# Attention scores as four 64x64 TensorE tiles of two head pairs, with thirds-wise loads, in a fused attention and mixture-of-experts kernel

## The reference

```python
# q, k, v: (4 batches, 8 heads, 576 positions, 64)
scores = scale * np.matmul(q, k.transpose(0, 1, 3, 2))
mask = (rel >= 0) & (rel < 64)                 # rel = query position - key position
attn = softmax(np.where(mask, scores, -1e9))   # with 1e-09 added to the sum
x = np.matmul(attn, v)                         # rows: 2304 tokens x 512

x = ((x @ w1) * (x @ w2)) @ w3 @ w_out         # 512 -> 1024 -> 1024 -> 512

e_idx = argmax(x @ w_gate)                     # one of 8 experts per token
out[mask] = gate_w * sigmoid(x @ w_output_gate)[e] * (relu(x @ ew1[e]) @ ew2[e])
```

## Time and profile before

| | |
|---|---|
| Three timed runs | 757.87, 755.08, 758.03 us (median 757.87) |
| The profiled execution | 755.37 us, its span 753.6 us |
| TensorE busy / its weight loads | 722.7 us (96%) / 663.5 us (88%) |
| VectorE, ScalarE, GpSimd busy | 326.3 (43%), 297.9 (40%), 122.0 us (16%) |
| DMA | 80.08 MB in 64187 packets, 23501 of them under 512 B |

### The profile page before, as it was taken

How to read it: one execution, slowest core, us unless ns; L and a number is a source line. 1 busy time by engine, 2 the same in 40 slices (tenths; PEclk the granted TensorE clock), 3 DMA queues, 4 the chain that set the end, 5 groups by cost and what they waited for, 6 DMA issues and landing times.

```text
span 753.6 us, 14552 instructions
## 1 busy us (share of the span) xinstructions
PE 722.7 (96%) x4832; PEld 663.5 (88%) x4833; DVE 326.3 (43%) x641; ACT 297.9 (40%) x720; POOL 122.0 (16%) x191
## 2 busy tenths in 40 slices
PE   5999999999999999999999994999999999999994
PEld 5999999999999999999999994888888888888883
DVE  3577445412144524442221276736265544652120
ACT  3577444422045434443211242335345544542211
POOL 7012011200011111111000001112222221222111
PEclk9999999999999999999999996999999999999998
DMA  9985212420012241205101043446265654411110
GB/s 300 232 261 164 75 33 62 118 70 1 29 47 60 60 130 33 60 29 197 70 1 43 1 182 112 144 149 200 95 206 194 235 181 135 166 33 42 31 42 29
DMA packets 64187, 80.08 MB, mean 106 GB/s; under 512 B 23501, under 2 KB 43981, under 8 KB 64144
## 3 DMA queue, kind: packets, MB, share of 16 engines
q1 hardware_dynamic: 59104, 64.01, 27.6%
q0 software_dynamic: 5040, 15.47, 5.9%
HBM read 70.03 MB, written 10.49 MB: 107 GB/s over the span
## 4 chain that ended last, share of the span: by engine, by line
PE 93%; DVE 3%; DMA 1%; ACT 1%; issue 1%; POOL 0%; POOLq 0%; ACTq 0%; DVEq 0%
PE bank L428 26%; PE bank L430 25%; PE bank L429 25%; PE bank L478 5%; PE bank L499 3%; PE bank L598 2%; PE bank L488 2%; PE bank L578 1%; DMA xs<-x_rows,gid 1%; DVE wbuf L901 1%; PE bank L440 1%; PE bank L570 0%; PE bank L466 0%; PE bank L462 0%; DMA w3r<-in_w3T 0%
## 5 line engine op out<-in xcount | busy, mean ns | idle before, releaser
L428 PE MATMUL bank<-Wh,abh 128*128 128x272 f32 (+1 forms) x288 | 83.8, 291 | 0.0
L430 PE MATMUL bank<-Wh,abl 128*128 128x272 f32 (+1 forms) x288 | 82.1, 285 | 0.0
L429 PE MATMUL bank<-Wl,abh 128*128 128x272 f32 (+1 forms) x288 | 81.8, 284 | 0.0
L650 ACT ACTIVATE prob<-prob,nmx 128x128 f32<-128x128 f32 x144 | 56.3, 392 | 63.7 <-DVE nmx L820 63.7
L901 DVE TENSOR_TENSOR wbuf<-raw,wbuf 128x1024 f32 (+1 forms) x64 | 75.4, 1221 | 11.9 <-ACT wbuf L715 11.7
L1144 POOL TENSOR_TENSOR prob<-prob,rec 128x384 f32<-128x384 f32 x48 | 39.8, 828 | 217.8 <-DVE rec L830 217.8
L428 PE MATMUL bank<-wbuf,xsTh 128*128 (+1 forms) x176 | 71.6, 407 | 2.3 <-DVE xsTl L1008 2.3
L428 PE MATMUL bank<-wbuf,hTh 128*128 x176 | 70.8, 402 | 0.0
L1053 DVE TENSOR_TENSOR hTl<-bank,hTh 128x512 fp32r<-128x512 f32 x44 | 28.4, 686 | 97.9 <-ACT hTh L763 97.9
L910 DVE TENSOR_TENSOR ab_f<-bank,a_sb 128x384 f32<-128x384 f32 x48 | 26.8, 558 | 98.8 <-PE bank L430 98.8
L430 PE MATMUL bank<-wbuf,xsTl 128*128 (+1 forms) x176 | 69.4, 395 | 0.0
(11 more groups left out here) (180 smaller groups left out, 1536.3 us busy)
## 6 DMA issues: line engine op xcount, KB each, us to landing
raw<-in_expert_w SPq DMA_DIRECT2D x64, 512.0 KB, 4.5
qbd<-in_qT SPq DMA_DIRECT2D x32, 144.0 KB, 3.6
kT<-in_kT SPq DMA_DIRECT2D x16, 288.0 KB, 3.9
x_rows<-x_sb POOLq DMA_DIRECT2D x18, 256.0 KB, 2.3
w3r<-in_w3T SPq DMA_DIRECT2D x8, 512.0 KB, 3.9
vA<-in_v SPq DMA_DIRECT2D x16, 256.0 KB, 3.1
vB<-in_v SPq DMA_DIRECT2D x16, 256.0 KB, 3.6
wo<-in_w_out SPq DMA_DIRECT2D x8, 256.0 KB, 6.7
```

Source lines behind the costliest of these rows:

```text
L428: pe.matmul(dst, lh, rh, start=first, stop=False)
L429: pe.matmul(dst, lh, rl, start=False, stop=False)
L430: return pe.matmul(dst, ll, rh, start=False, stop=last)
L650: ex_i = act.activation(prob[k % 4][:, cols], prob[k % 4][:, cols], ACT.Exp, bias=nmx[:, row], accum_out=sums[:, row])
```

## The change

1. **Scores.** `qbd` goes. `qT` and `kT` hold two head pairs (r = 0, 1) side by side on the free axis; the partitions hold the two heads (h = 0, 1) of a pair. For each block, four products of 64 rows x 64 columns x 128 keys are issued: (h, r) = (0,0), (0,1), (1,0), (1,1). h picks the half of the array's rows (and a bank: 4 or 7), r the half of its columns (the half of the bank's partitions). A group is now three blocks of head h of both pairs, and the groups of one h = 0 and one h = 1 are made together: scores are issued at even k alone, 12 matmuls for two groups.
2. **The product with v** goes to bank 6 always, and waits for `o_lo >= G` instead of `G - 1`.
3. **Loads** come by thirds (three blocks) of two head pairs, into one set of buffers, each waiting for the step that frees that third; the two memsets of `qbd` and the wait for them go.
4. **w1 and w2**: pieces are split at the fold's steps 4, 6, 8, 10, 11, 12, 13, 14; their rows, and v, are laid out in another order before the launch, to fit the new order of the heads. `group_cols` follows.

```diff
-        qbd = [put(f"qbd{i}", NBLK * P) for i in range(2)]
-        kT = [put(f"kT{i}", S) for i in range(2)]
-        vA = [put(f"vA{i}", SFULL * P) for i in range(2)]
-        vB = [put(f"vB{i}", SFULL * P) for i in range(2)]
+        qT, kT = put("qT", 2 * S), put("kT", 2 * S)
+        vA, vB = put("vA", 2 * SFULL * P), put("vB", 2 * SFULL * P)
...
+        step_of = lambda k: (k // (2 * NGRP), k % (2 * NGRP) // 2, k % 2)
+        score_bank = lambda h: bank[4 + 3 * h]
...
-        w12_steps = [3, 4, 5] + list(range(6, len(w_order), 2))
+        w12_steps = [4, 6, 8] + list(range(10, len(w_order) - 1))
...
+            def load_qk(u, j):
+                cols = slice(j * 3 * WIN, (j + 1) * 3 * WIN)
+                for t, src in ((qT, qT_in), (kT, kT_in)):
+                    sp.dma_start(t[:, :].rearrange("p (r s) -> p r s", s=S)[:, :, cols],
+                                 src[bass.ds(u * 2, 2), :, cols].rearrange("r p s -> p r s")).then_inc(qk_in[j], 16)
...
+            def next_qk(u, j):
+                sp.wait_ge(s_done, u * (2 * NGRP) - (2 * NGRP) + min(2 * j + 4, 2 * NGRP))
+                load_qk(u, j)
+
+            def next_v(u, j):
+                sp.wait_ge(o_done, u * (2 * NGRP) - (2 * NGRP) + 2 * j + 2)
+                load_v(u, j)
...
-            with sp.Fori(PAIRS // 2, UNITS // 2) as n:
-                for r in range(2):
-                    next_qk(n * 2 + r, r)
-                    next_v(n * 2 + r, r)
+            with sp.Fori(2, UNITS // 2) as u:
+                next_qk(u, 0)
+                next_v(u, 0)
+                next_qk(u, 1)
+                next_qk(u, 2)
+                next_v(u, 1)
+                next_v(u, 2)
...
-                if k < NG:
-                    r, j = k // NGRP % 2, k % NGRP
-                    if j == 0:
-                        pe.wait_ge(qk_in[r], (b * (PAIRS // 2) + (k // (2 * NGRP) + 1)) * (16 * 3))
+                if k < NG and k % 2 == 0:
+                    u, j, _ = step_of(k)
+                    pe.wait_ge(qk_in[j], (b * (PAIRS // 2) + u + 1) * (16 * 2))
                     pe.wait_ge(masked, G + 1)
                     for i in range(3 * j, 3 * j + 3):
-                        mm = pe.matmul(bank[4][:, (i % 3) * P:(i % 3 + 1) * P], qbd[r][:, i * P:(i + 1) * P],
-                                       kT[r][:, key_start(i):key_start(i) + P], start=True, stop=True)
-                    mm.then_inc(s_done, 1)
+                        for h in range(2):
+                            rows = slice(h * D, (h + 1) * D)
+                            for r in range(2):
+                                mm = pe.matmul(score_bank(h)[r * WIN:(r + 1) * WIN, (i % 3) * P:(i % 3 + 1) * P],
+                                               qT[rows, r * S + i * WIN:r * S + (i + 1) * WIN],
+                                               kT[rows, r * S + key_start(i):r * S + key_start(i) + P], start=True, stop=True)
+                            if i % 3 == 2:
+                                mm.then_inc(s_done, 1)
...
-                    pe.wait_ge(o_lo, G - 1)
+                    pe.wait_ge(o_lo, G)
                     for i in range(3):
-                        vt = v_tile(r, 3 * j + i)
-                        for h in range(2):
-                            mm = pe.matmul(bank[6 + k % 2][h * D:(h + 1) * D, i * WIN:(i + 1) * WIN], vt[:, h * D:(h + 1) * D],
+                        for r in range(2):
+                            mm = pe.matmul(bank[6][r * D:(r + 1) * D, i * WIN:(i + 1) * WIN], v_tile(r, 3 * j + i)[:, h * D:(h + 1) * D],
...
-            then(pool.memset(qbd[0][:, :], 0.0))
-            then(pool.memset(qbd[1][:, :], 0.0))
-            pool.sem_inc(qbd_zero, 1)
```

More of the change, by code:

```diff
@@ L196, in build @@
         w12_hi, w12_lo = sem("w12_hi"), sem("w12_lo")
-        qbd_zero = sem("qbd_zero")
-        qk_in, v_in_ok = [sem("qk_in0"), sem("qk_in1")], [sem("v_in0"), sem("v_in1")]
+        qk_in, v_in_ok = [sem(f"qk_in{j}") for j in range(NGRP)], [sem(f"v_in{j}") for j in range(NGRP)]
         s_done, masked, nmx_ok, exp_ok = sem("s_done"), sem("masked"), sem("nmx_ok"), sem("exp_ok")
@@ L226, in v_tile @@
         def v_tile(r, i):
-            t = (vA if key_start(i) % P == 0 else vB)[r]
-            c = key_start(i) // P
+            t = vA if key_start(i) % P == 0 else vB
+            c = key_start(i) // P * 2 + r
             return t[:, c * P:(c + 1) * P]
+        v_tiles = [[sorted({key_start(i) // P for i in range(3 * j, 3 * j + 3) if key_start(i) % P == odd * WIN})
+                    for j in range(NGRP)] for odd in range(2)]
+        step_of = lambda k: (k // (2 * NGRP), k % (2 * NGRP) // 2, k % 2)
+        score_bank = lambda h: bank[4 + 3 * h]
         def for_chunks(chunk):
@@ L353, in _ @@
                 load_wo(1, i)
-            def load_qk(u, r):
-                for h in range(2):
[L357 to L375, removed]
@@ L384, in _ @@
+            load_w3(4)
+            load_v(0, 2)
             load_w12(1)
-            load_w3(4)
+            next_qk(1, 0)
+            load_w3(5)
             load_w12(2)
-            load_w3(5)
+            next_v(1, 0)
+            next_qk(1, 1)
+            next_qk(1, 2)
             load_w12(3)
-            next_qk(2, 0)
-            next_v(2, 0)
+            load_w3(6)
+            next_v(1, 1)
             load_w12(4)
-            load_w3(6)
-            next_qk(3, 1)
             load_w12(5)
@@ L660, in attend_end @@
                     act.wait_ge(o_done, G - 1)
-                    act.activation(xTh[:, group_cols(k - 2, parity)], bank[6 + k % 2][:, 0:3 * WIN], ACT.Copy).then_inc(o_hi, 1)
+                    act.activation(xTh[:, group_cols(k - 2, parity)], bank[6][:, 0:3 * WIN], ACT.Copy).then_inc(o_hi, 1)
             def hi_w3(it):
@@ L835, in attend_end @@
                     dve.wait_ge(o_hi, b * NG + k - 1)
-                    dve.tensor_tensor(xTl[:, cols], bank[6 + k % 2][:, 0:3 * WIN], f32(xTh[:, cols]), ALU.subtract).then_inc(o_lo, 1)
+                    dve.tensor_tensor(xTl[:, cols], bank[6][:, 0:3 * WIN], f32(xTh[:, cols]), ALU.subtract).then_inc(o_lo, 1)
             def lo_w3(it):
@@ L1220 @@
     by_pair = lambda a: a.reshape(B * H // 2, 2, S, D)
+    by_rows = lambda w: w.reshape(H // 4, 2, 2, D, -1).transpose(0, 2, 1, 3, 4).reshape(w.shape)
     laid = {
@@ L1223 @@
         "kT": by_pair(k).transpose(0, 1, 3, 2).reshape(-1, 2 * D, S),
-        "v": by_pair(v).transpose(0, 2, 1, 3).reshape(-1, S, 2 * D),
-        "w1": inputs["moe_w1"],
-        "w2": inputs["moe_w2"],
+        "v": v.reshape(B * H // 4, 4, S, D).transpose(0, 2, 1, 3).reshape(-1, S, 4 * D),
+        "w1": by_rows(inputs["moe_w1"]),
+        "w2": by_rows(inputs["moe_w2"]),
         "w3T": w3.reshape(-1, P, nj, P).transpose(0, 3, 2, 1).reshape(-1, P, nj * P),
```

31 lines of the change are left out of this document (19 added, 12 removed).

## The result

The change is faster, by 1.1%. Four runs took 748.33, 748.32, 748.13 and 747.51 us (median 748.23), against a median of 756.86 for the kernel before in the same comparison: ratio 0.9886, 95% interval 0.9861 to 0.991. The forecast was 747.5, in a range of 742 to 764. The profiled execution took 748.33 us with a span of 746.6, where before it was 755.37 and 753.6.

A forecast was written before the change was run, and what follows sets the result against it. TensorE, busy 96% of the span and 93% of the chain of waits, was taken to bound the kernel. -15.2 + 4.85 + 3.0 - 1.1 = -8.45 us from 755.37 gave 746.9, forecast as 747.5, range 742 to 764.

The forecast's parts named there:

- A: Attention's scores: four quarters work at once, 0.67 us for two groups instead of 2 x 0.66; 15.2 us saved over 23 pairs.
- B: Changes of tile shape around the scores at even k: 0.15 to 0.20 us each added, 4.85 us lost in all.
- C: End of each batch: with one bank the second product with v waits for the first's reading, 0.75 us each, 3.0 lost.
- D: First pair of groups: made together, no wait for bank 4, own work starts at about 26.86 instead of 27.98; -1.1 us.
- off the path: Memsets, loads by thirds, splits of w1 and w2, VectorE and ScalarE: all hidden beside TensorE, zero us.
- two-at-a-time rival: Scores: row halves take turns, so packing saves nothing; +6.75 us, 762.1 us, slower; chance 0.20.
- partly packed one: Rival on the scores: a pass every 0.042 us, 7.6 us saved, 754.5 us, no change that counts; chance 0.15.
- what is late next: After the first pair's scores, the step's g1_lo (VectorE, done at 26.80) sets own work's start at about 26.86.
- late-load rival: Thirds late by 0.35 us at each of 24 even steps cancel the gain (755 us), by 0.6, 761; chance 0.03.
- Not packed at all: Rival on the scores: no quarters overlap, 2.66 us a pair, +37 us, 793 us; chance 0.02.

The follow-up runs named there:

- e4: The change with the three blocks (six passes) of one quarter issued in a row, then the next quarter; 766.11 us (one run).
- e5: The change with transposes and product with v swapped at k = 3, 5, 7, 9, one more change of shape in 16 gaps; 751.45 us.
- e8: The change with the product with v also made for two groups at once, at odd k alone, one copy and one subtraction for both; 742.99 us.
- e1: The change with the product with v of a batch's last group in bank 7, waiting for o_lo as before the change; 745.4 us.
- e7: The change with every third of q and k asked for only when the whole set is free; 753.25 us.
- e11: e8 with w3's sixth piece asked for right behind the fifth in SyncE's order; 743.58 us.
- e12: The change with scores issued by quarters, two blocks (four passes) each, then block 2 for each quarter; 748.2 us (one run).
- e3: The change with a block's four tiles in the order (h, r) = (0,0), (1,0), (0,1), (1,1); 748.54 us (one run).
- e10: e7 with w3's sixth piece asked for ahead of the late third of q and k; 749.87 us.
- e9: e8 with ScalarE's and VectorE's splits of w1, w2 and w3 put behind the next step's exponentials; 750.78 us.

## Why the prediction was right, and where it was not

| term | forecast | measured |
|---|---|---|
| A and B, scores and changes of shape | -10.35 | -11.2 |
| C, one bank | +3.0 | +3.3 |
| D, the first pair | -1.1 | -0.7 |
| off the path | 0 | +0.2, and the first scores 0.16 later |
| attention's part | -8.45 | -8.3 |
| behind it | 0 | +1.1 |

**A was right in mechanism and size.** The row of 64-column tiles was the right one to go by: a pass every 0.028 us was asked for and came. The two-at-a-time rival fell with L489's stretch (0.82, not 1.5), and the partly packed one with it: 24 passes in 0.64 us are six full rounds of about 0.11. (The pass that just pays for the rival's 6.75 us is 0.043 us, not 0.044 as the prediction has it.) The Trainium skill, TensorE: Matmul & The Clock Gate, section Packing small matmuls, has 3.07 times for four row tiles, of another shape (32 rows, 512 columns). Here four quarters gave four times a single quarter's pace: one pass per 0.11 us in e4's first quarter, four in the change. For this shape the measurement decides.

**B was right in its unit** (0.15 in the scores' stretches, 0.816 less 0.67; e5: 0.14 per change) **and counted slightly high.** The scores' own stretches came out at -12.0, against -15.2 plus 23 times 0.15, -11.7. Of the rest of B, 1.4 us at k = 0 and 2, 1.2 was seen: 0.14 to 0.20 in the transposes' stretch at each k = 2, and 0.21 in the own work ahead of two of the three k = 0. At the third it was 0.01: TensorE stands idle for 0.63 us ahead of those scores in both kernels, and the change of shape fits in. The other stretches of transposes and own work are 0.3 shorter in sum, mostly by 0.01 to 0.03 each. What TensorEngine Tiling (Array Packing) in the Trainium skill says under Key Properties, that a change of mode drains TensorE, agrees with the gaps read here: the loads stand idle for 0.17 us ahead of the product with v 44 times, before and after. The Trainium skill gives no time there; e5 has 0.14 us for one change more, e8 0.34 for one way in and out less.

**C was right** in place, count and cause; it was sized at 0.75 us each and is 0.83 (e1). It was read off the end of the batch before, where ScalarE and VectorE already did this very work.

**D was right about what was late next only for the next 3 us.** Own work starts at 26.82, as forecast (26.86). But the step is then too short for what hangs on VectorE: the group's reciprocal is done at 29.5, GpSimd runs from 29.60 to 30.43, and the transposes behind the step wait. The change's timeline there:

```profile
26.82 0.19 PEld L437 LDWEIGHTS bank<-xTh,w3h 128*128 128x128 f32 x1 [0.79 <-issue]
...
29.60 0.83 POOL L1153 TENSOR_TENSOR prob<-prob,rec 128x384 f32<-128x384 f32 x1 [14.95 <-DVE rec L842]
...
30.48 0.31 PEld L501 LDWEIGHTS bank<-ident,prob 128*128 128x128 f32 x3 [0.59 <-POOL prob L1153]
```

So 1.3 us were gained and 0.64 given back. The step that failed is "what is late next", asked once where it had to be asked again one wait further on.

**"All zero" off the path was too flat a statement for the fold.** In the change it cost only 0.2 us, but e7 to e11 show how thin the cover is: w3's pieces already landed 1 to 2 us later than ScalarE could have taken them, and the 3.5 us by which e7 asked for one later became 4.2 us of TensorE, 1.4 of them by the clock. The late-load rival had the size right (e7), and the wrong load. The thirds themselves had more in hand than the prediction read: after the scores of k = 2 the first is asked for, due at k = 6; after those of k = 4 the other two, due at k = 8 and 10. That is four to six steps, not two to four; e7 left the first one two, and still no score waited for it.

**The rivals belong to other orders of the loops.** "Not packed at all" was put at 24 x 0.11, and I expected it of e4. Even with each quarter's passes in a row TensorE overlaps two quarters, 1.62 us, and e4's 766 us is near what I gave the two-at-a-time case (762). That case was real, then, but not for the order that the change has.

**The end at 747.5** against 748.2 is partly luck: +1.1 us behind attention was forecast by nothing and goes with the length of the clock's low stretch, and the median before came out at 756.9, so that the gain by medians is 8.6 us where the two profiled executions differ by 7.0.

## What to carry to other kernels

Four 64x64 tiles run at once if all four quarters get work within a few passes of each other: make the quarter the inner loop, and then count the changes of shape (0.14 to 0.20 us each), which took more than a quarter of what packing gained (4.2 us of 15.4); e8 avoided others by putting work of one shape side by side. When a buffer is halved, read the one place where its two users follow each other directly. When loads share one queue in order, a wait in front of a load is paid by everything behind it, so the load to watch is not the one moved but the next big one behind it. And where TensorE is kept idle for 2 to 3 us, it can cost half as much again or more behind that, by the clock (1.4 us behind 2.8 in e7, 1.5 behind 2.0 in e11).

## What the runs showed of the hardware that I had not expected

- TensorE starts passes of another quarter ahead of earlier ones of a busy quarter: in e4 the second quarter's first load starts at 0.275 us, when the first has started four of its six; four passes in a row for a quarter (e12) cost 0.02 us, six cost 0.27.
- Row halves in turn (e3) or column halves in turn (the change) are the same, 0.82 us.
- w3's pieces of 512 KB took from about 4 to 7 us from asking to use in the fold: 5.0 in the change (39.13 to 44.17), 5.2 in e7, 6.8 in e10 (48.78 to 55.59) and 7.1 in e11 (46.57 to 53.70), where ScalarE waited for the landing each time. What else is in flight differs; which of it does this was not tried.
- The clock's low stretch around the end of the routing is 13.7 or 17.1 us long, whichever the kernel (five and nine of 14 profiled executions), and some 0.85 us of the kernel's end go with it. What decides its length was not tried.
- In the fold the clock fell to 1.2 GHz for 3.4 us in e7, e9 and e11, each time at the end of an idle stretch of TensorE or up to 1.1 us behind it (2.8 us idle in e7, 1.7 in e9, 2.0 in e11). In e10 TensorE was idle for 1.7 us and the clock did not fall.
